# Retention and two MLPs on one core: the masked quarter of each chunk left out, and first tiles loaded in parts

## The reference

```
scores = q @ k.T / sqrt(64)              # 8 batches, 8 heads, 576 positions, 64 wide
x = (scores * gamma_h ** (i - j), 0 where j > i) @ v     # heads side by side: 4608 x 512
x = max(x @ w1, x @ w2, x @ w3) @ w_out                  # 512 -> 768 -> 512
x = ((x @ u1) * (x @ u2)) @ u3 @ u_out                   # 512 -> 1024 -> 1024 -> 512
```

## Time and profile before

| | |
|---|---|
| median of 3 runs | 1220.27 us (1220.11 to 1221.44) |
| the profiled execution | 1221.08 us, its span in the trace 1219.2 us |
| TensorE busy | 1209.0 us, 99% |
| VectorE, ScalarE, GpSimd busy | 739.5, 487.5, 431.8 us |
| DMA | 169.55 MB, mean 139 GB/s |

### The profile page before, as it was taken

The page is one execution under the profiler, slowest core; times in us unless marked ns, Lnnn a source line. Parts: engine busy times, 40 slices in busy tenths (PEclk is TensorE's granted clock), DMA queues, the critical chain, the costliest instruction groups (busy, mean ns, idle before and its releaser), DMA issues.

```text
span 1219.2 us, 21648 instructions
## 1 busy us (share of the span) xinstructions
PE 1209.0 (99%) x8594; PEld 1190.1 (98%) x8594; DVE 739.5 (61%) x1065; ACT 487.5 (40%) x781; POOL 431.8 (35%) x234
## 2 busy tenths in 40 slices
PE   8999999999999999999999999999999999999999
PEld 8898899999999999999999999999999999999998
DVE  5555747746454454658887777454545456876652
ACT  3444544423232322326655444232424234554451
POOL 3645645220202010063787660202020217465550
PEclk9999999999999999999999999999999999999999
DMA  9999943021212030234554541313121252444441
GB/s 346 332 364 376 322 141 134 33 85 46 78 46 85 26 105 27 73 136 147 179 218 170 169 139 53 110 52 110 60 104 64 99 189 89 155 157 161 162 156 65
DMA packets 87332, 169.55 MB, mean 139 GB/s; under 512 B 9272, under 2 KB 58680, under 8 KB 87232
## 3 DMA queue, kind: packets, MB, share of 16 engines
q1 hardware_dynamic: 87232, 168.17, 39.2%
HBM read 106.27 MB, written 61.87 MB: 138 GB/s over the span
## 4 chain that ended last, share of the span: by engine, by line
PE 92%; DMA 3%; SPq 2%; DVE 1%; issue 1%; ACT 0%; POOL 0%; ACTq 0%; DVEq 0%; POOLq 0%
PE ps L1268 28%; PE ps L1270 28%; PE ps L1269 28%; PE ps L1177 2%; PE ps L1120 1%; PE ps L1192 1%; PE ps L1165 1%; PE ps L1194 1%; PE ps L1196 1%; PE ps L1140 1%; DMA vs<-vv 1%; DMA qks<-qk 1%; DMA xd<-xst 1%; DMA hd<-h 1%; DVE probs L952 0%
## 5 line engine op out<-in xcount | busy, mean ns | idle before, releaser
L1268 PE MATMUL ps<-chi,whi 128*128 128x384 f32 x2016 | 673.9, 334 | 0.9 <-ACT w L931 0.6
L1270 PE MATMUL ps<-chi,wlo 128*128 128x384 f32 x2016 | 673.5, 334 | 0.0
L1269 PE MATMUL ps<-clo,whi 128*128 128x384 f32 x2016 | 673.4, 334 | 0.0
L674 POOL TENSOR_TENSOR raw<-raw,raw 128x768 f32<-128x768 f32 (+3 forms) x102 | 267.8, 2646 | 582.7 <-DMA raw<-xd 203.6
L1268 PEld LDWEIGHTS ps<-chi,whi 128*128 128x128 f32 x2016 | 378.4, 188 | 2.1 <-ACT w L931 1.0
L1269 PEld LDWEIGHTS ps<-clo,whi 128*128 128x128 f32 x2016 | 378.5, 188 | 0.0
L1270 PEld LDWEIGHTS ps<-chi,wlo 128*128 128x128 f32 x2016 | 378.4, 188 | 0.0
L940 DVE TENSOR_TENSOR clo<-raw,chi 128x768 fp32r<-128x768 f32 (+2 forms) x168 | 253.2, 1535 | 29.6 <-ACT chi L851 29.5
L851 ACT CAST chi<-raw 128x768 fp32r<-128x768 f32 (+2 forms) x168 | 180.3, 1081 | 83.8 <-PE ps L1270 54.7
L931 ACT COPY w<-ps 128x384 f32<-128x384 f32 x126 | 60.6, 481 | 240.6 <-PE ps L1270 239.0
L918 ACT COPY u<-ps 128x384 f32<-128x384 f32 x126 | 60.6, 481 | 160.6 <-PE ps L1270 159.0
(11 more groups left out here) (61 smaller groups left out, 796.0 us busy)
## 6 DMA issues: line engine op xcount, KB each, us to landing
gd<-h SPq DMA_DIRECT2D x96, 192.0 KB, 1.9
raw<-gd SPq DMA_DIRECT2D x24, 768.0 KB, 6.4
qks<-qk SPq DMA_DIRECT2D x30, 576.0 KB, 7.4
hd<-h SPq DMA_DIRECT2D x72, 192.0 KB, 1.9
raw<-hd SPq DMA_DIRECT2D x24, 576.0 KB, 6.0
x2d<-h SPq DMA_DIRECT2D x48, 192.0 KB, 2.2
raw<-x2d SPq DMA_DIRECT2D x24, 384.0 KB, 4.2
outT<-h SPq DMA_DIRECT2D x48, 192.0 KB, 1.9
```

What stands on the lines that cost most here:

```text
L674: return nc.gpsimd.tensor_tensor(out_, a, b, op)
L1268: nc.tensor.matmul(to, w1, x1, start=(start and k == 0), stop=False, skip_group_check=True)
L1269: nc.tensor.matmul(to, w1, x2, start=False, stop=False, skip_group_check=True)
L1270: last = nc.tensor.matmul(to, w2, x1, start=False, stop=(k == KH[st] - 1), skip_group_check=True)
```

## The change

**Scores and values.** Of the 128 by 128 scores of a chunk, the quarter with keys in the second half and queries in the first is all masked. The new kernel computes scores in two products per head and chunk: the first 64 keys with 128 queries and the second 64 keys with the last 64 queries. From step 2 on (`SINGLE = 2`) two pairs are interleaved (`scores_of_two`), so that their products lie in the four quadrants of the array; for that, odd pairs have the two halves of their keys exchanged (`key_rows`), in the inputs too. The tail has 64 keys now instead of 128. The values likewise: `values_of_halves` takes the first 64 queries with the first 64 keys, and the tails; `values` takes the last 64 queries with all 128 keys. The tail's values get a tile `vtail` of their own, and the memsets of unused halves go.

**Order.** In every step from 1 on it is now: scores, quarters, `query_states`, `values_of_halves`, `values`, `sum_state`. SUMS_FIRST is gone. From step 2, VectorE decays head 0 of both pairs and then head 1 of both; `query_states` waits for head 0 only, and for head 1 ahead of its last chunk (`decayed_heads`). `scores_of_two` waits for rows and `x_out` of both pairs at its start.

**First tiles.** For the first tile of C, the second stage, the blocks 0 and 3 are loaded where all four were and 6 and 2 an iteration later. For that of I, the third, the load comes earlier in iteration 64, ahead of one store, and waits block by block on the splits of the tile before (`I_OVER`).

The diff, without lines that only rename or lay out buffers:

```diff
--- before.py
+++ after.py
@@ -167,6 +166,9 @@
+I_OVER = {0: 0, 3: 2, 6: 4, 2: 1}
@@ -183,6 +185,8 @@
+RAW_OF = {_tau: _a for _a, _tau in RAW_AT.items()}
@@ -190,7 +194,17 @@
-SUMS_FIRST = (4, 5)
+SINGLE = 2
...
+def key_rows(n, half):
+    return slice((half ^ n % 2) * DH, (half ^ n % 2) * DH + DH)
...
+def decayed_heads(m, all_heads):
+    return min(3 * NP, 6 * m + (4 if all_heads else 3 if m < SINGLE else 2))
@@ -450,19 +464,17 @@
             def load_v(n):
-                sp.dma_start(vs[:, n % 6, 0:NC * CH], vv[n, :, :]).then_inc(v_loaded[v_sem(n)], 16)
+                sp.dma_start(vs[:, n % 6, :], vv[n, :, :]).then_inc(v_loaded[v_sem(n)], 16)
...
-                sp.dma_start(vs[:, n % 6:n % 6 + 2, 0:NC * CH], vv[n:n + 2, :, :].rearrange("n p c -> p n c")
+                sp.dma_start(vs[:, n % 6:n % 6 + 2, :], vv[n:n + 2, :, :].rearrange("n p c -> p n c")
...
-                n = 2 * m
-                sp.dma_start(vs[TAIL:P, n % 6:n % 6 + 2, NC * CH:], vt[n:n + 2, :, :].rearrange("n p c -> p n c")
-                             ).then_inc(vt_loaded[m % 3], 16)
+                sp.dma_start(vtail[:, m % 3, :], vt[m, :, :]).then_inc(vt_loaded[m % 3], 16)
@@ -537,7 +549,9 @@
                             sp.wait_ge(stored[i][j], 16 * groups_through(tau - TILES))
-                if t == 0:
+                if t == 0 and st == I:
+                    sp.wait_ge(combined, 4 * tau)
+                elif t == 0:
@@ -546,6 +560,8 @@
                 for pos in blocks:
+                    if t == 0 and st == I:
+                        sp.wait_ge(c_lo, 7 * (tau - 1) + I_OVER[pos] + 1)
@@ -640,6 +656,8 @@
                             load_raw(tau, (0, 3, 6, 2) if tau // TILES == C else (0, 3, 2))
+                        if it == 64:
+                            load_raw(I * TILES)
@@ -659,10 +677,12 @@
                     store(it, 0, 0)
-                if it == 64:
-                    load_raw(I * TILES)
-                if tau is not None and not two_parts and not at_once:
+                if tau == C * TILES:
+                    load_raw(tau, (0, 3))
+                elif tau is not None and not two_parts and not at_once:
...
+                if it == RAW_OF[C * TILES] + 1:
+                    load_raw(C * TILES, (6, 2))
@@ -706,6 +726,8 @@
                         pool.wait_ge(w_lo, 2 * FIRST_W[C] - 1)
+                    if tau == I * TILES:
+                        pool.wait_ge(c_lo, 7 * (tau - 1) + 4)
@@ -948,26 +970,24 @@
                     dve.wait_ge(valued, n - 3)
-                for h in range(2):
-                    nc.vector.tensor_tensor(
-                        probs[n % 4][:, h, 0:NC * CH].rearrange("p (n c) -> p n c", c=CH),
-                        ps[:, 2 * (n % 2) + h, :].rearrange("p (n c) -> p n c", c=CH),
-                        dec[:, p // 2, p % 2, h, :].unsqueeze(1).broadcast_to([P, NC, CH]), ALU.mult
-                    ).then_inc(decayed, 1)
+                nc.vector.tensor_tensor(
+                    probs[n % 4][:, h, 0:NC * CH].rearrange("p (n c) -> p n c", c=CH),
+                    ps[:, 2 * (n % 2) + h, :].rearrange("p (n c) -> p n c", c=CH),
+                    dec[:, p // 2, p % 2, h, :].unsqueeze(1).broadcast_to([P, NC, CH]), ALU.mult
+                ).then_inc(decayed, 1)
...
+                rows = key_rows(n, 1)
...
-                    probs[n % 4][TAIL:P, :, NC * CH:SEQ],
-                    ps[TAIL:P, S_TAIL[0]:S_TAIL[1] + 1, (n % 2) * TAIL:(n % 2 + 1) * TAIL],
-                    dec[TAIL:P, p // 2, p % 2, :, TAIL:CH], ALU.mult).then_inc(decayed, 1)
+                    probs[n % 4][rows, :, NC * CH:SEQ],
+                    ps[rows, S_TAIL[0]:S_TAIL[1] + 1, (n % 2) * TAIL:(n % 2 + 1) * TAIL],
+                    dec[rows, p // 2, p % 2, :, TAIL:CH], ALU.mult).then_inc(decayed, 1)
...
-                if n in SUMS_FIRST:
-                    dve.wait_ge(queried, n - 1)
@@ -1005,17 +1026,18 @@
             nc.vector.memset(idle[:, :], 0.0).then_inc(idle_zeroed, 1)
-            for i in range(4):
-                nc.vector.memset(probs[i][0:TAIL, :, NC * CH:SEQ], 0.0).then_inc(zeroed, 1)
-            for i in range(6):
-                nc.vector.memset(vs[0:TAIL, i, NC * CH:], 0.0).then_inc(zeroed, 1)
-            dve.wait_ge(zeroed, 10)
...
-                for n in made_in(m):
-                    decay_scores(n)
-                    if n == 0:
-                        mask_decay()
-                        make_state(n)
+                if m < SINGLE:
+                    for n in made_in(m):
+                        decay_scores(n, 0)
+                        decay_scores(n, 1)
+                        if n == 0:
+                            mask_decay()
+                            make_state(n)
+                else:
+                    for h in range(2):
+                        for n in made_in(m):
+                            decay_scores(n, h)
@@ -1105,27 +1127,49 @@
+            def scores_of(n, c, half, first_query):
+                for h in range(2):
+                    own = slice(h * DH, h * DH + DH)
+                    keys = SEQ + c * CH + half * DH
+                    nc.tensor.matmul(ps[key_rows(n, half), 2 * (n % 2) + h, c * CH + first_query:(c + 1) * CH],
+                                     rows_of(n)[own, keys:keys + DH],
+                                     rows_of(n)[own, c * CH + first_query:(c + 1) * CH],
+                                     start=(c == 0), stop=(c == NC - 1), skip_group_check=True)
...
+            def tail_scores(n):
+                for h in range(2):
+                    own = slice(h * DH, h * DH + DH)
+                    last = nc.tensor.matmul(ps[key_rows(n, 1), S_TAIL[h], (n % 2) * TAIL:(n % 2 + 1) * TAIL],
+                                            rows_of(n)[own, KQ_COLS - TAIL:KQ_COLS], rows_of(n)[own, SEQ - TAIL:SEQ],
+                                            start=True, stop=True, skip_group_check=True)
+                last.then_inc(scored, 1)
...
-                if n >= 4:
-                    pe.wait_ge(x_out, n - 3)
...
-                    for h in range(2):
-                        own = slice(h * DH, h * DH + DH)
-                        keys = SEQ + c * CH
-                        nc.tensor.matmul(ps[:, 2 * (n % 2) + h, c * CH:(c + 1) * CH], rows_of(n)[own, keys:keys + CH],
-                                         rows_of(n)[own, c * CH:(c + 1) * CH],
-                                         start=(c == 0), stop=(c == NC - 1), skip_group_check=True)
-                for h in range(2):
-                    own = slice(h * DH, h * DH + DH)
-                    last = nc.tensor.matmul(ps[:, S_TAIL[h], (n % 2) * TAIL:(n % 2 + 1) * TAIL],
-                                            rows_of(n)[own, KQ_COLS - CH:KQ_COLS], rows_of(n)[own, SEQ - TAIL:SEQ],
-                                            start=True, stop=True, skip_group_check=True)
-                last.then_inc(scored, 1)
+                    for half in range(2):
+                        scores_of(n, c, half, 0)
+                tail_scores(n)
...
+            def scores_of_two(first):
+                pair = (first, first + 1)
+                for n in pair:
+                    pe.wait_ge(qk_loaded[rows_sem(n)], rows_count(n))
+                pe.wait_ge(decayed, 3 * first)
+                pe.wait_ge(x_out, first - 2)
+                for c in range(NC):
+                    for half in range(2):
+                        for n in pair:
+                            scores_of(n, c, half, half * DH)
+                for n in pair:
+                    tail_scores(n)
@@ -1156,8 +1200,10 @@
                     pe.wait_ge(x_out, n - 1)
-                pe.wait_ge(decayed, min(3 * (first + 2) + 4, 3 * NP))
+                pe.wait_ge(decayed, decayed_heads(first // 2 + 1, False))
...
+                    if c == NC:
+                        pe.wait_ge(decayed, decayed_heads(first // 2 + 1, True))
@@ -1168,15 +1214,36 @@
+            def values_of_halves(first):
+                pair = (first, first + 1)
+                pe.wait_ge(decayed, 3 * (first + 2))
...
+                pe.wait_ge(queried, first + 2)
+                pe.wait_ge(vt_loaded[first // 2 % 3], 16 * (first // 6 + 1))
+                for c in range(NC):
+                    for n in pair:
+                        rows = key_rows(n, 0)
+                        for h in range(2):
+                            nc.tensor.matmul(ps[out_rows(n, h), 2 * (n % 2), c * CH:c * CH + DH],
+                                             vs[rows, n % 6, c * P + h * DH:c * P + h * DH + DH],
+                                             probs[n % 4][rows, h, c * CH:c * CH + DH],
+                                             start=False, stop=False, skip_group_check=True)
+                for n in pair:
+                    rows = key_rows(n, 1)
+                    for h in range(2):
+                        nc.tensor.matmul(ps[out_rows(n, h), 2 * (n % 2) + 1, 0:TAIL],
```

(66 more changed lines are left out.)

## The result

The changed kernel takes 1249.37 us (median of 4 runs, 1247.78 to 1251.97), the one before 1220.48: ratio 1.0238, 95% interval 1.0216 to 1.0259. I had forecast 1212.8 and faster. It is slower by 29 us.

What follows compares the result with a forecast made beforehand. TensorE and the DMA engines were both taken as full, DMA becoming the bound. Gains of 0, 4.1 + 1.7 and 1.7 us made 7.5 off the 1219.2 us span: 1211.7, median 1212.8; eight-in-ten range 1205 to 1218.

Steps and rivals of the forecast that it cites:

- Rival C: Retention: loads start later, engines never get fuller, saved TensorE time becomes waits for `qks`; 1218.6 us, chance 0.11.
- Rival D: Retention: keys land too late, so `sum_state` waits and steps lengthen; slower, 1224.6 us, chance 0.05.
- The quads: Scores and values: four quadrant products side by side cost 0.11 us with 128 moving columns, about 0.056 with 64.
- Rival B: Scores and values: in a run, a 64-column quad costs 0.11 us like a 128-column one; 1218.3 us, chance 0.06.
- the stretch from `query_states` to the halves: Each step: `query_states` without the drain behind it was put at 0.82 us.
- the prediction's upper bound: TensorE's matmul savings over 14 steps of scores and 16 of values, 18.2 us in all.
- The 4.1 us of fuller engines: Loads from 50 to 145 us come 4.1 us sooner if DMA engines hold a 1.05 share instead of 1.005.
- The end of the retention: Once no urgent loads remain, step 15 saves 1.23 us and the last values 0.49, together 1.7.
- The first 50 us: Early retention steps: 4.2 us saved in matmuls against 3 to 5 lost in waits, so no gain.
- the wait that I had listed: Steps 2 to 4: `make_state` delays the decays with little to cover it; TensorE waits some 2 us in each.
- The copies of x (b): `scores_of_two` wants both `x_out`; the second copy ends 0.8 us behind the values, covered by 0.93 us of state sums.
- The edits to the first tiles: Loading the first tiles of C and I differently gains nothing, with 0.8 us of waits as upper bound.

Runs made afterwards that it cites:

- light changed kernel: The changed kernel with loads of rows, keys and values from pair 6 on cut to 8 of 128 partitions (results not the reference's): 1218.32 us.
- scores only: The changed kernel with the values again as before, keeping the new scores, tails and order: 1232.37 us, ratio 1.0086.
- additions: The kernel before plus 32 tiny products (128 instructions) a step ahead of every `query_states`: 1255.89 us with full loads, 1236.77 with cut loads.

## Why the prediction was wrong
**What bounds the kernel.** I named two full resources, TensorE and the DMA engines, and reasoned which of them would bind. The one that did was a third, TensorE's supply of instructions, which both share in: more instructions per us on one side, a longer queue ahead of each packet on the other. This is the step that failed: with the loads cut the same changed kernel takes 31 us less. No term of the sum had a price per instruction, although the change adds 128 to a step of 312, and the wait that shows it stood in the view of the waits. Rival C had "the loads start later"; it is data that it meant, and its 1218.6 is nearly as far off as the forecast. Rival D, the only slower one, did not occur: `sum_state` never waited for keys.

**TensorE's own time.** The quads were right: scores start to quarters in 90.40 - 88.78 = 1.62 us (forecast 1.64), `values_of_halves` 95.25 - 94.51 = 0.74 with its drain (0.72). Rival B does not hold for four quadrants side by side: the 32 products of `values_of_halves` start within 101.17 - 100.68 = 0.49 us, 0.015 us each. Nor do the 25 ns from start to start that the Trainium skill gives as the least ("TensorE: Matmul & The Clock Gate", section "Wait — 56ns, not 53.3ns?"). Mis-sized was the stretch from `query_states` to the halves, 1.16 us for 0.82: TensorE waits there for its own `queried`, 0.16 us of it shown as a wait, which before had other work behind it. With it, and the sums at 1.08, query, values and sums take 3.96 us where they took 3.99: the halves of the values win nothing. A step saves 0.78 instead of 1.23 (light changed kernel). Over 14 steps that is 11 us where the prediction's upper bound had 18.2.

**The DMA side.** The 4.1 us of fuller engines never came into play; the share fell to 88% instead of rising to 1.05. The end of the retention, put at 1.7 us of gain, gave none even with the loads cut (21.05 us for 20.76).

**The first 50 us, put at no gain.** They were a loss: step 5 starts at 63.8 us instead of 50.7. In the 13 are the order's 5 (`make_state` uncovered, the wait that I had listed and set off against savings) and refill gaps of 3.9, 2.1 and 4.1 with the lower clock behind them, less what the new products save; the parts are not told apart further.

**The copies of x (b), put at nothing.** 6.0 us here and 9.9 with scores only. The copies themselves wait 10.9 us in the changed kernel for their stores, 2.4 before (ScalarE's waits); the stores stand in SP's order behind keys that wait for the sums, 61.2 us in all in SP's waits and 19.8 before.

**The clock.** Not in the prediction. At 26.55 us, behind the gap of 3.6 us, the 64 records of the scores take 2.84 us:

```profile
21.18 0.69 PE L1184 MATMUL ps<-vdec,ks_first 128*64 128x64 f32 x17
25.50 1.12 PE L1184 MATMUL ps<-vdec,ks_first 128*64 128x64 f32 x15 [3.62 <-issue]
...
26.55 2.84 PE L1135 MATMUL ps<-qks 64*64 64x128 f32 x64
```

They take 1.57 at the full clock. The lower level held for 23.9 us in five stretches, each begun by a gap of about 4 us (three of them) or by a wait and a refill gap close together; the gap of 2.1 us at 47.3 us did not bring it. The waits grew by 29.5 us and the retention by 29.8, so the matmuls saved (14 x 0.78 = 11) and the clock's cost about cancel; 23.9 us at half speed cannot cost more than 12. That is a sum, not an experiment.

**The edits to the first tiles** were rightly put at nothing.

## What to carry to other kernels
Count instructions of the busiest engine per us, not only its array time: here the kernels with 440 a step got 256 in 6.4 to 6.7 us while the DMA engines were full, and in 5.2 (changed kernel) and 5.9 us (additions) with the loads cut, and cutting a product in two halves, where it doubles weight loads and products, is paid from that. A wait put down to "issue" is worth numbering: if its instruction stands at a fixed place modulo the block, a change that uses instructions faster can meet it at any block edge, as this one did. And moving one group later in an in-order step moves what other engines and queues do behind it; the order was worth testing by itself before anything was built on it.

## What the runs showed of the hardware
TensorE's instructions come in packets of 16 KB, 256 instructions, through the same DMA engines as the data. The packet started 1 to 8 us after the block before was entered with the data loads full (3.4 on average in the changed kernel, 2.3 in the one before), 0 to 3 us (1.3) with them cut; in the three gaps of the table its block's first instruction ran 2.3 to 2.4 us after its start. So a block needs 3.6 to 10.3 us to come here, and TensorE stands still when it has used up the one before sooner. The Trainium skill, "Runtime: NRT & Kernel Launch", section "Instruction fetch mechanics", describes refill in blocks of 256 instructions, and the numbering agrees; it calls the cost of crossing into a new block mostly hidden, and for the changed kernel the measurement decides otherwise: 25.5 us in thirteen crossings.

Four weight loads and four products of 64 rows by 64 columns, one for each quadrant, run at 0.06 us a set, for the eight sets of `values_of_halves` in a row. With 2 moving columns instead of 64 a set costs the same: the 16 sets of the additions take 89.52 - 88.56 = 0.96 us.
